# Another order of steps, other banks for the key-value products, and fewer fillers in a linear-attention and MoE kernel

## The reference

```
# 1: linear attention with complex decay, for each batch, head and time t
mag = sqrt(a_re^2 + a_im^2);  scale = min(mag, 0.999) / (mag + 1e-6)
S = (a_re + i a_im) * scale * S + k v^T        # 48 x 48 state
y[t] = q[t] @ Re(S)
# 2: rmsnorm and a gated layer, d = 384, f = 1536
xn = y / sqrt(mean(y^2) + 1e-6) * rms_g
x = (silu(xn @ w_gate) * (xn @ w_val)) @ w_out
# 3: top-1 mixture of 8 experts, f = 1024: logits from x / |x| and the normed expert
#    embeddings, softmax, relu(x @ w1[e]) @ w2[e], times the gate
```

## Time and profile before

| | |
|---|---|
| median of 3 runs | 1305.21 us (1304.82 to 1309.6) |
| profiled execution | 1303.45 us, its span 1301.7 us |
| tensor engine busy | 1203.5 us, 92% of the span |
| VectorE, ScalarE, GpSimd busy | 766.8, 600.7, 366.4 us |
| ahead of the first turn of pass 0 | 34.0 us |
| first turn of pass 1, 2 and 3 | 113.3, 184.1, 255.7 us |
| end of the first part | about 974 us |

### The profile page before, as it was taken

One profiled execution on the slowest core, in us unless ns is written; L12 is line 12 of the kernel. 1 busy time (PEld: TensorE's weight loads), 2 busy tenths in 40 slices (PEclk: granted clock), 3 DMA queues, 4 the chain that ended last, 5 costly groups with the idle time before them and its releaser, 6 DMA issues. The chain is left out here.

```text
span 1301.7 us, 46434 instructions
## 1 busy us (share of the span) xinstructions
PE 1203.5 (92%) x20081; PEld 1041.7 (80%) x20081; DVE 766.8 (59%) x1549; ACT 600.7 (46%) x1293; POOL 366.4 (28%) x361
## 2 busy tenths in 40 slices
PE   1788999999999999999999999999978999999996
PEld 0556787879687887878687887878857999999996
DVE  5696847485767658484667557263117555555553
ACT  3646354545546554646455554434222344333442
POOL 8506051323333150413333150200003122222221
PEclk9899999999999999999999999999997999999998
DMA  7142011111202020111111020000005634333410
GB/s 206 26 123 59 7 39 40 39 40 33 45 15 57 9 58 20 38 40 39 39 30 42 9 45 10 15 15 3 13 13 161 209 127 143 132 134 131 137 37 30
DMA packets 151845, 78.36 MB, mean 60 GB/s; under 512 B 130715, under 2 KB 144571, under 8 KB 151664
## 3 DMA queue, kind: packets, MB, share of 16 engines
q1 hardware_dynamic: 143264, 59.04, 17.0%
q0 software_dynamic: 4384, 11.88, 3.1%
q10 hardware_dynamic: 4016, 4.73, 1.0%
HBM read 66.15 MB, written 11.06 MB: 59 GB/s over the span
## 5 line engine op out<-in xcount | busy, mean ns | idle before, releaser
L887 PE MATMUL pO<-wo_sb,hid 128*128 128x384 f32 x576 | 206.9, 496 | 4.0 <-issue 2.8
L572 DVE TENSOR_TENSOR hid<-silu,pGV 128x256 f32<-128x256 f32 x144 | 60.0, 417 | 177.2 <-ACT silu L711 177.2
L887 PEld LDWEIGHTS pO<-wo_sb,hid 128*128 128x128 f32 x576 | 102.6, 191 | 58.6 <-issue 5.2
L873 PE MATMUL pGV<-xT_hi,wg_hi 128*128 128x256 f32 x432 | 139.4, 323 | 6.1 <-DVE hid L572 6.1
L711 ACT ACTIVATE silu<-pGV 128x256 f32<-128x256 f32 x144 | 55.4, 385 | 181.1 <-PE pGV L875 178.9
L1198 ACT ACTIVATE h_hi<-pH 128x256 fp32r<-128x256 f32 x128 | 49.1, 385 | 164.9 <-PE pH L1143 164.9
L875 PE MATMUL pGV<-xT_hi,wg_lo 128*128 128x256 f32 x432 | 122.4, 283 | 1.0 <-issue 1.0
L874 PE MATMUL pGV<-xT_lo,wg_hi 128*128 128x256 f32 x432 | 122.0, 282 | 0.0
L873 PE MATMUL pGV<-xT_hi,wv_hi 128*128 128x256 f32 x432 | 121.5, 281 | 0.0
L874 PE MATMUL pGV<-xT_lo,wv_hi 128*128 128x256 f32 x432 | 121.5, 281 | 0.0
L875 PE MATMUL pGV<-xT_hi,wv_lo 128*128 128x256 f32 x432 | 121.2, 281 | 0.0
(11 more groups left out here) (213 smaller groups left out, 3043.9 us busy)
## 6 DMA issues: line engine op xcount, KB each, us to landing
w_sb<-in_moe_w SPq DMA_DIRECT2D x18, 1536.0 KB, 10.5
re<-in_a_re SPq DMA_DIRECT2D x24, 192.0 KB, 2.9
im<-in_a_im SPq DMA_DIRECT2D x24, 192.0 KB, 3.7
qin<-in_q SPq DMA_DIRECT2D x24, 192.0 KB, 2.8
kin<-in_k SPq DMA_DIRECT2D x24, 192.0 KB, 3.6
vin<-in_v SPq DMA_DIRECT2D x24, 192.0 KB, 3.3
routed_rows<-x ACTq DMA_DIRECT2D x24, 192.0 KB, 2.0
wo_sb<-in_moe_w_out SPq DMA_DIRECT2D x1, 2304.0 KB, 9.5
```

The lines of the kernel that those rows point to most:

```text
L572: w.tensor_tensor(hid[:, f, :], act_g[f % 2], pGV[f % 2][:, TOKS:2 * TOKS], ALU.mult).then_inc(sm["h_ready"], 1)
L873: mm.matmul(to, hi, x_hi[:, kk, :], start=(kk == 0), stop=False)
L887: ins = mm.matmul(pO[:, 0:HD], hid[:, f, s_ * P:(s_ + 1) * P], wo_sb[:, f, :], start=(f == 0), stop=(f == NF - 1))
```

## The change

The diff below has its core; code that only moves between lines is cut.

- **The list.** `STEPS` is reordered. Turns 0 and 1 stand ahead of the roots. The norm stands behind the sums. The turn of the rows in (`turn_in`) stands behind level 0. Gates come in pairs behind a level: 0 and 1, 2 and 3, 4 and 5, 6 alone, 7 and 8, 9 alone, 10 and 11. Phases 0 and 1 and `own` 0 come a level sooner. Both `turn_back` stand side by side, then gate 9. Squares and abs stand around gate 11, and outputs 2 and 3 come last. Weight splits 0 and 1 stand in the turns, 2, 3 and 4 in the levels, 5 behind them.
- **Sums of squares.** They are a step of their own, `ssq`, in the next pass behind turn 3, and write to `x2[u]` in place of the phases' tile.
- **Key-value products.** A new step, `products`, makes those of both units one behind the other, ahead of the outputs, in the banks `pG[u]` in place of `pM`. Level 0 then waits for the state of the pass before.
- **Fillers.** One in place of an out (before two), two in place of each gate (before three for gates 0 to 4, one for the rest).
- **Constants.** VectorE clears `A`. ScalarE makes the mask copies, as a step `masks` behind the first roots. The common wait ahead of pass 0 goes.
- **Loads.** SP issues values with the first two turns of a pass, then the next queries and keys, then the decays of the pass after the next, with waits for both units at once. The load of `w_out` comes behind the second decays, queries and keys.

```diff
-BUSY_TURNS, BUSY_LEVELS, BUSY_END = 2, 3, 1
+BUSY_TURNS, BUSY_LEVELS = 1, 2
 STEPS = [
-    ("glu", "norm", 0), ("pre", "roots", 0), ("pre", "roots", 1), ("lev", "turn", 0), ("lev", "turn", 1), ("fin", "out", 0), ("fin", "out", 1),
-    ("lev", "turn", 2), ("lev", "turn", 3), ("pre", "sums", 0), ("pre", "sums", 1), ("fin", "out", 2),
+    ("lev", "turn", 0), ("lev", "turn", 1), ("pre", "roots", 0), ("pre", "roots", 1), ("fin", "out", 0), ("fin", "out", 1),
+    ("lev", "turn", 2), ("lev", "turn", 3), ("glu", "ssq", 0), ("glu", "ssq", 1), ("pre", "sums", 0), ("pre", "sums", 1), ("glu", "norm", 0), ("fin", "out", 2),
...
+    ("lev", "level", 0), ("fin", "out", 7), ("fin", "out", 8), ("glu", "turn_in", 0),
+    ("lev", "level", 1), ("pre", "double", 0), ("pre", "double", 1), ("fin", "out", 9), ("fin", "out", 10), ("fin", "out", 11),
+    ("wts", "split", 2), ("lev", "level", 2), ("pre", "angle", 0), ("fin", "square", 1), ("glu", "gate", 0), ("glu", "gate", 1),
+    ("lev", "level", 3), ("pre", "angle", 1), ("pre", "phase", 0), ("fin", "route", 0), ("glu", "gate", 2), ("glu", "gate", 3),
+    ("wts", "split", 3), ("lev", "level", 4), ("pre", "phase", 1), ("glu", "gate", 4), ("glu", "gate", 5),
+    ("lev", "level", 5), ("pre", "own", 0), ("glu", "gate", 6),
+    ("wts", "split", 4), ("lev", "level", 6), ("fin", "logits", 0), ("glu", "gate", 7), ("pre", "rotate", 0), ("pre", "own", 1), ("glu", "gate", 8),
+    ("lev", "turn_back", 0), ("lev", "turn_back", 1), ("pre", "rotate", 1), ("glu", "gate", 9), ("wts", "split", 5),
+    ("lev", "products", 0), ("lev", "products", 1), ("lev", "output", 0), ("lev", "output", 1), ("glu", "gate", 10), ("lev", "state", 0), ("sq", "squares", 0),
+    ("sq", "squares", 1), ("sq", "abs", 0), ("glu", "gate", 11), ("sq", "abs", 1),
+    ("lev", "output", 2), ("lev", "output", 3), ("lev", "state", 1),
...
                     for n in range(2 * KC):
                         if n == 2:
-                            decays(0, 1)
-                            queries_and_keys(0, 1)
+                            sp.wait_ge(sm["ima_ready"], U)
+                            sp.wait_ge(sm["absre_ready"], U)
+                            decays(1)
+                            sp.wait_ge(sm["kcs_ready"], U + CREDIT)
+                            queries_and_keys(1)
+                            sp.dma_start(wo_sb[:, :, :], w_out.rearrange("(f p) d -> p f d", p=P)).then_inc(sm["wo_loaded"], 16)
...
+                    for i in range(NP):
+                        n0 = i * U
+                        if i > 0:
+                            sp.wait_ge(sm["tp_ready"], i * TA + TA + 2)
+                            values(i)
+                        if 0 < i < NP - 1:
+                            sp.wait_ge(sm["kcs_ready"], n0 + U + CREDIT)
+                            queries_and_keys(i + 1)
+                        if i < NP - 2:
+                            sp.wait_ge(sm["ima_ready"], n0 + 2 * U)
+                            sp.wait_ge(sm["absre_ready"], n0 + 2 * U)
+                            decays(i + 2)
...
-                    for u in range(U):
-                        done(g.memset(A[u][:, :, :], 0.0))
...
+                    for u in range(U):
+                        w.memset(A[u][:, :, :], 0.0).then_inc(sm["a_cleared"], 1)
...
-                                w.scalar_tensor_tensor(out=state[:, :, :], in0=pM[0:D2, 0:HD].rearrange("p (h d) -> p h d", h=H),
+                                w.scalar_tensor_tensor(out=state[:, :, :], in0=pG[u][0:D2, 0:HD].rearrange("p (h d) -> p h d", h=H),
...
+                            elif step == "ssq":
+                                u = x
+                                act.wait_ge(sm["x_ready"], m * U + u + 1 + ONE)
+                                s.activation(x2[u][:, :], xs[u], ACT.Square, accum_out=ssq[:, u:u + 1]).then_inc(sm["ssq_ready"], 1)
+                                act.wait_ge(sm["ssq_ready"], m * U + u + 1)
...
-                            elif step == "state":
+                            elif step == "products":
                                 u = x
                                 pe.wait_ge(sm["evac_done"], i * TA + CREDIT + TF + 2 + 2 * u)
-                                pe.wait_ge(sm["x_ready"], n0 + u + 1 + ONE)
+                                pe.wait_ge(v_loaded[u], (i + 1) * 16)
+                                pe.wait_ge(a_high[u], (i + 1) * A_COPIES + ONE)
                                 for h in range(H):
                                     for j in range(D2 // BLOCK):
                                         at = slice(j * BLOCK, (j + 1) * BLOCK)
-                                        ins = mm.matmul(pM[at, h * D:(h + 1) * D], KTM[u][:, h, at], v_t[u][:, h, :], start=True, stop=True)
+                                        ins = mm.matmul(pG[u][at, h * D:(h + 1) * D], KTM[u][:, h, at], v_t[u][:, h, :], start=True, stop=True)
                                 ins.then_inc(sm["kv_ready"], 1)
```

More of the change, by code:

```diff
@@ L98 @@
-    ("lev", "turn_back", 1), ("pre", "rotate", 1), ("glu", "gate", 6),
-    ("lev", "output", 0), ("lev", "output", 1), ("glu", "gate", 7),
-    ("lev", "state", 0), ("glu", "gate", 8), ("sq", "squares", 0), ("sq", "squares", 1), ("glu", "gate", 9),
-    ("lev", "output", 2), ("lev", "output", 3), ("glu", "gate", 10), ("sq", "abs", 0), ("sq", "abs", 1), ("glu", "gate", 11),
-    ("lev", "state", 1),
+    ("lev", "turn", 10), ("lev", "turn", 11), ("lev", "first", 1), ("pre", "quotients", 1), ("wts", "split", 1), ("fin", "out", 6), ("glu", "scale", 0),
@@ L749, in body @@
                             if stage not in stages:
-                                if "lev" in stages and "fin" not in stages and step in ("gate", "out"):
-                                    busy(BUSY_TURNS if step == "out" else BUSY_LEVELS if x < 5 else BUSY_END)
+                                if "lev" in stages and step in ("gate", "out"):
+                                    busy(BUSY_TURNS if step == "out" else BUSY_LEVELS)
                                 continue
```

99 lines of the change are left out of this document (33 added, 66 removed).

## The result

The changed kernel is slower: 1315.52 us (median of 7 executions, 1312.04 to 1319.08) against 1305.21 us (7 executions, 1302.95 to 1309.6), a ratio of 1.0074 with a 95% interval of 1.0051 to 1.0098. The forecast was 1290.0 us, with a range up to 1306. The profiled executions took 1312.04 and 1303.45 us.

The account below looks back on a forecast made before the run. Passes from 1 on were taken as bound by the tensor engine's work plus few waits, pass 0 by chains over ScalarE, VectorE and GpSimd. -7.0 - 8.5 + 1.0 = -14.5 from 1303.45 gave 1289.0 profiled, median 1290, range 1275 to 1306.

Parts of the forecast that it names:

- Waits between levels and hidden rows: Passes 2 to 11: tensor waits for masked copies (8.8 us) and hidden rows (4.9 us) both go, -13.7 us.
- Changes of kind and products: Passes 2 to 11: paired gates save 0.9 us a pass, products side by side and beside the outputs 0.2.
- turns back: Passes 2 to 11: third group of transposes waits for the first one's evacuation, +0.6 us a pass.
- The turn from one pass to the next: Passes 2 to 10: ScalarE's late queue and the norm's root delay turns 6 and 7, +1.3 us a pass (0 to 3).
- Bursts: All passes: tensor waits with no visible releaser in runs of short instructions, +1.0 us (-8 to +12).
- Loads: Same bytes in another order, weight tiles of pass 0 asked for earlier beside VectorE's work; no effect on time.
- Start: Ahead of pass 0: memsets move to VectorE, GpSimd's first product stays at about 16.5 us; +0.5 us (0 to +1).
- Pass 0, first turn of pass 1 at 106: End of pass 0: levels end at 95.7 us, first turn of pass 1 starts at 106 against 113.3.
- behind them rotation 0 can start 6 us earlier, since its phase is done: Pass 0, behind the levels: rotation 0 starts 6 us earlier, diag 1 comes at about 101 against 105.33.
- Fillers cost nothing in pass 0: Pass 0: fillers stand beside VectorE's work and cost nothing; in pass 1 they were in the way.
- the turn of the passes: Rival at the pass boundary: its cost exceeds all gains from 2.9 us a pass; 1312 at 3.8 us, chance 0.14.

Follow-up runs that it names:

- Experiment 1: Changed kernel with the norm moved from behind the sums to behind turns 6 and 7; 1309.0 us, ratio 1.0023 to the kernel before.
- experiment 6: Changed kernel with the norm behind turns 6 and 7, gate 10 between products and outputs 0 and 1, roots ahead of turns 0 and 1; 1293.9 us.
- Experiment 2: Changed kernel with gate 10 moved between the key-value products and outputs 0 and 1; 1303.5 us, ratio 0.9979 to the kernel before.
- experiment 11: Changed kernel with 16 small transposes more on the tensor engine ahead of its first pass; 1317.4 us, ratio 1.0088 to the kernel before.
- experiment 8: Changed kernel with loads of values, queries, keys and decays started behind the twelfth turn of a pass, not the second; 1324.9 us.
- experiment 7: Changed kernel with the edits of Experiment 1 and Experiment 2, plus own 0 and split 4 behind level 6; 1294.7 us.
- experiment 13: The kernel with the four edits, plus split 4 moved behind the turns back, beside split 5; 1294.5 us.
- experiment 14: The kernel of experiment 13, plus rotation 0 and own 1 moved behind the turns back in every queue; 1319.0 us.
- experiment 3: Changed kernel with the numbers of fillers of the kernel before in passes 0 and 1; 1321.8 us, ratio 1.0121 to the kernel before.
- experiment 10: The kernel with the four edits, without fillers at the places of gates 9, 10 and 11 in pass 0; 1295.3 us.
- the four edits: Changed kernel with norm behind turns 6 and 7, gate 10 ahead of outputs, roots ahead of turns, own 0 and split 4 behind level 6; 1292.5 us.

## Why the prediction was wrong, step by step

**Waits between levels and hidden rows, -13.7 us.** Right. Neither is left in passes 2 to 10.

**Changes of kind and products, -1.1 a pass; turns back, +0.6.** Right about the pairs and the turns back: the latter wait 3.1 / 9 = 0.34 us a pass, and both together take 1.8 us where they took 1.3. Gates without their waits take 27.1 us a pass where they took 28.3. Wrong about the products and outputs side by side, which took 5.3 us a pass without their waits, against 5.2; this is where the bursts come in.

**The turn from one pass to the next, +1.3 a pass.** The mechanism was right down to the norm's root (forecast at 8.5 us behind the first turn, in pass 3 at 268.89 - 259.98 = 8.9), and the term was mis-sized: 15.7 / 9 = 1.74 us. The mean square, forecast to be there at 8.2 us, took 0.95 us (0.15 before) and was there at 8.8. Experiment 1 took 1.1 of it away by moving the norm, experiment 6 the rest but for 0.1 by moving the roots. That is 4 us of the miss.

**Bursts, +1.0 over all passes.** This failed, as a mechanism priced at nearly nothing: waits without a releaser were 13.9 us in passes 2 to 10 against 10.0. They weren't just more of the same, they had moved into the block that the change created. Products, then outputs 0 and 1, make one run of 2 x 96 + 2 x 128 = 448 short instructions (96 matmuls of the products and 256 of all outputs in pass 3, each with its weight load). Places where instructions run out stand every 256, so a run of 448 always holds at least one, and often one with a full 256 of short instructions ahead of it. A run of 192 and one of 256 with a gate between them rarely do. Experiment 2 showed it by the exchange of one gate (-8.5 us of these waits, -12.0 us of time), and experiment 11 showed why a shift doesn't help: it moves the places, and the run is as long as before. The bounds of the term (-8 to +12) held it; the value I took stood too near nothing.

**Loads, nothing.** Not safe to leave out: experiment 8 puts a worth of 9.4 us on their place in the changed kernel's turns. In passes 2 to 10 6.4 us are waits without a releaser, longer with DMA traffic beside them. Whether the change gained or lost by its own move of the loads, from behind the quotients to the turns, wasn't tried and isn't shown.

**Start, +0.5 (0 to +1).** Right about the mechanism (GpSimd's first product at 16.58), 1.1 in size.

**Pass 0, first turn of pass 1 at 106.** Wrong by 10 us, the largest single miss: it was at 116.43. The forecast followed VectorE alone. Its timeline in pass 0 of the changed kernel, in the place of the earlier trace rows:

```profile
54.97 2.56 DVE L547 SCALAR_TENSOR_TENSOR wg_lo<-hid,gcol,wg_hi 128x1536 fp32r<-128x1536 f32 x1
...
62.65 1.48 DVE L508 TENSOR_TENSOR QT<-QT,RK 96x512 f32<-96x512 f32 x1
...
93.78 0.55 DVE L466 TENSOR_REDUCE diag<-qcs 128x8 f32<-128x384 f32 x1 [1.82 <-POOL qcs L368]
96.07 1.82 DVE L547 SCALAR_TENSOR_TENSOR wv_lo<-hid,gcol,wv_hi 128x1536 fp32r<-128x1536 f32 x1 [1.73 <-ACT wv_hi L685]
...
104.92 0.55 DVE L466 TENSOR_REDUCE diag<-qcs 128x8 f32<-128x384 f32 x1 [2.86 <-POOL qcs L368]
...
110.51 1.04 DVE L523 SCALAR_TENSOR_TENSOR state<-state,goes_on,PP 96x384 f32<-96x384 f32 x1 [2.93 <-PE pM L834]
```

The splits in the turns took 2.56 us each and not 1.8, level 0 began at 62.65 in place of 61.0, and two new waits stood between levels 5 and 6. The step that failed most is "behind them rotation 0 can start 6 us earlier, since its phase is done". The phase was done, and ScalarE wasn't free. Its timeline:

```profile
89.36 1.57 ACT L644 ACTIVATE A<-pG 32x256 f32<-32x256 f32 x4 [20.79 <-PE pG L793]
90.95 3.48 ACT L653 ACTIVATE A<-qcs 32x256 f32<-32x256 f32 x8
94.46 1.58 ACT L685 ACTIVATE wv_hi<-hid,gcol 128x1536 fp32r<-128x1536 f32 x1
96.06 1.07 ACT L644 ACTIVATE A<-pG 64x512 f32<-64x512 f32 x2
97.15 1.28 ACT L672 ACT_TABLE_LOAD   x1
98.44 0.52 ACT L672 ACTIVATE cs<-mag 128x384 f32<-128x384 f32 x1
```

It worked from 89.36 without a pause, so rotation 0 began on GpSimd only at 100.10, and diag 1 came at 104.92 in place of 101. On the tensor engine the turns back, the fillers behind them and the products then ran at the lower clock:

```profile
99.14 2.92 PE L814 MATMUL pT<-ident,KT 96*128 96x96 f32 x16 [3.11 <-DVE KT L510]
101.85 2.82 PE L733 MATMUL pO<-ident,upto 128*128 128x384 f32 x4
104.60 2.29 PE L846 MATMUL pG<-vin,RK 128*32 128x48 f32 x96
```

Four matmuls of fillers take 2.82 us here and 1.46 at full clock. The state then waited for these outputs (2.93 us). Experiments 7, 13 and 14 show that no one of the chains is the sole bound: each edit removed or shortened the wait that it was aimed at, and others grew; pass 0 changed by -0.7, -0.4 and +2.3 us, about as little as by a shift alone (0.9 and 1.9). What a lower clock by itself costs there wasn't measured; 13.6 us more of it in passes 0 and 1 are at most 6.8 us, if all of that time were tensor work on the path.

**Fillers cost nothing in pass 0.** Perhaps wrong by little: with 10 more of them pass 0 is 2.4 us longer (experiment 3), without the last six it is 1.4 shorter (experiment 10), both near the spread of that pass. That fewer are a gain in pass 1 was right: forecast 175.6 - 106 = 69.6 us, measured 69.3.

**Sum.** Of the 23 us between the forecast of 1289.0 for the profiled execution and 1312.04, the first turn of pass 1 holds 10.4. In passes 2 to 10, forecast at -5.1 plus some of the burst term and measured at +4.4, it's another 9 to 10: 4.0 of the norm's queue, about 3 of the waits without a releaser, and the rest spread over outs and turns, where it wasn't traced further. Pass 11 and the rest were forecast at -1.9 and gave 0. The second part adds 2.5 by the spread between executions. Among the rivals the one with the right mechanism was the turn of the passes; it was put at 2.9 us a pass or more to decide, and measured 1.74. The kernel ended slower since three terms of 3 to 10 us went the same way.

## What to carry to other kernels

When steps are reordered, follow each queue on its own from the moved step to the end of the stretch. Here "its input is ready sooner" was true for the rotation, and its engine had 8 us of other work in front of it.

A long run of short matmuls is a cost of its own on the tensor engine, though none of its instructions is slow: put one block of long matmuls between two short ones, and compare the waits without a releaser before and after. An exchange of one step was worth 12 us here.

When one operation waits in a queue for another engine (the norm's root), place it where the waiting is behind all that the bounding engine needs next; the order with the four edits took the changed kernel's idea from 0.7% slower to 0.9% faster.

## What the runs showed of the hardware

Tensor waits without a releaser stand at whole multiples of 256 instructions, moved with 32 instructions put in front, and one of them grew from 0.16 to 1.92 us when the DMA engines carried 149 GB/s ahead of it. That DMA traffic makes them longer rests on two such pairs, the sum of experiment 8 and the count over sixteen traces (0.89 against 0.17 us); traffic alone wasn't tried.

The same mark, no releaser, can stand on a wait of another kind: in experiment 14 the tensor engine waited for VectorE's rows, as its start 0.10 us behind their end shows eight times.

Beside GpSimd's products VectorE slowed by more than I had counted, and not only in operations with two inputs: the mean square of two numbers a partition took 0.95 us, a split of a weight tile 2.56 or 2.6 us against 1.80, and the first operation on the state 2.15 against 0.61.
